# A load order in a fused attention and feed-forward kernel: the second batch's keys ahead of the third tile's queries

## The chip, the cores and the metric

The kernel runs on one core of a Trainium2 chip (trn2). The metric is the device time of one execution in microseconds (us). Before the change it is 861.98 us, the median of 3 runs (861.78 to 862.18).

The engines of the core are named as in the profile: PE is the matrix engine (PEld its weight loads), DVE the vector engine, ACT the scalar engine, POOL the GpSimd engine, and SP the engine that in this kernel issues every DMA. The engines run their own instruction streams and wait for each other through semaphores. SPq in a row is the time in which SP's sequencer issues a DMA; the transfer itself then runs on the core's 16 DMA engines.

## The reference

Three stages follow each other: attention over pooled keys and values, a gated feed-forward layer with RMS normalization, and a second feed-forward layer.

```python
# q, k, v: batch 4, heads 8, sequence 576, head_dim 64
k_p = k.reshape(B, H, Sp, 8, D).mean(axis=3)          # Sp = 576 / 8 = 72
v_p = v.reshape(B, H, Sp, 8, D).mean(axis=3)
scores = (1 / sqrt(D)) * q @ k_p^T
attn = softmax(scores)
x = (attn @ v_p), heads side by side                  # 2304 tokens x 512
xn = x / sqrt(mean(x * x) + 1e-6) * rms_g
h = silu(xn @ w_gate) * (xn @ w_val)                  # 512 x 1536 each
y = h @ w_out                                         # 1536 x 512
z = silu(y @ w2_in) @ w2_out                          # 512 x 2048, 2048 x 512
```

## The kernel before

The 2304 tokens are 18 tiles of 128. The attention stage goes through them one by one; it ends in the profile at about 90 us. The rest of the time belongs to the two feed-forward layers, whose products are built from split operands; the change touches nothing there.

Keys and values of one batch (8 heads, 72 pooled positions each, so 576 rows) are loaded whole, pooled by sums of 8 and then used by the four or five tiles of that batch. The batches begin in tiles 0, 4, 9 and 13. Queries are loaded tile by tile.

Names that the change and the prediction touch:

- `load_kv(b, kind)` (line 526) issues the load of batch b's keys (kind 0) or values (kind 1) into the buffer `kv`. For b = 1, kind 0 it waits for nothing and issues two DMAs: four chunks of 128 rows (L545, 1024 KB) and the last 64 rows (L547, 128 KB). Below these are k1 and k1's tail; v0 and v1 are the values of batches 0 and 1. A part of v1 goes out first (L536).
- `load_q(n)` (line 549) issues the load of tile n's queries into `qs[:, n % 2]` (L554, 256 KB, in pieces of 64 numbers). From n = 2 on it first waits until PE has transposed tile n - 2, whose buffer it takes. Below, q0, q1, q2, ... are these loads and tiles.
- `load_q(1)` stands inside `load_kv(0, 1)`, and `load_q(4)` inside `load_kv(1, 1)`.
- The vector `gT` (L697) holds rms_g; it is first used when tile 0 is normalized.

On PE, a list (`order`) written out by rules sets the sequence. In its step s it holds scores(s) (L1900), the transpose of the probabilities of tile s - 1 (prT, L1912), the transpose of the queries of tile s + 1 (L1887), from step 4 on the transpose of a finished x tile (L1944), where a batch begins with tile s + 1 the transpose of that batch's keys (L1878), and at last probabilities times values for tile s - 1 (pv, L1931). PE takes them strictly in that order: what waits holds all that is behind it.

The other engines feed it: POOL pools keys and values from batch 1 on (L830, L834, then L839 for keys into `ktwice`), DVE takes the maximum and subtracts it (L1478, L1483) and divides (L1505), ACT copies transposes out of PSUM (L1402 for queries, L1411 for probabilities, L1385 for keys) and takes exponentials (L1077). The transposed keys and the transposed probabilities share one region of PSUM, so the keys' transpose also waits until ACT has copied the probabilities of the tile before:

```python
def transpose_k(b):
    if b >= 1:
        pe.wait_ge(s_kTc, b)
    if first_tile[b] >= 1:
        pe.wait_ge(s_pTc, first_tile[b] - 1)
```

Before the attention PE does 30 transposes of an identity matrix (L2145), whose results nobody uses.

Of the kernel before, what the change touches and what calls it, by code (L numbers as in the profile page):

```python
# [20 lines left out]
def ffn_kernel(nc, q, k, v, w_gate, w_val, w_out, rms_g, w2_in, w2_out, out):  # L21
# [26 lines left out]
    def parts(n):  # L48
        at, found = n * P, []
        while at < (n + 1) * P:  # L50
            b = at // S
            end = min((b + 1) * S, (n + 1) * P)
            found.append((b, at - n * P, end - at))
            at = end
        return found
# [34 lines left out]
    for ph, (ffn, p) in enumerate(PHASES):  # L90
# [10 lines left out]
        if ph in ENDINGS:  # L101
# [26 lines left out]
                (BX, 1, 1, False), (BY, 2, 6, False), (BZ, 6, 2, False)]  # L128

    XORDER = [fx for _, _, fx, _ in PRODUCTS]  # L130

    def form_count(b, f):
# [50 lines left out]
    def esum(e, what, t):  # L183
# [3 lines left out]

    EHOME = [0, 1, 2, 0, 1, 3, 0]
    pieces = [EPART if fw < 3 else 1 for _, fw, _, _ in EPRODUCTS]
    e_load = [[16 * sum(pieces[m] * (e + (m <= i)) for m in range(NF) if EHOME[m] == EHOME[i]) for i in range(NF)]  # L190
              for e in range(2)]
# [14 lines left out]
    made += [("b", j) for j in range(2 * PART)]  # L206
    FOLD_AT = {("unit", first_unit[1] + 1 + j): ("b", j) for j in range(2 * PART)}
    f_pieces = [PART if fw < 3 else 1 for _, fw, _, _ in WPRODUCTS]
    f_load = [[16 * sum(f_pieces[m] * (e + (m <= i)) for m in range(i % 3, NF, 3)) for i in range(NF)] for e in range(2)]
    U2, N2 = first_unit[2], last_down[1] + 1  # L210
# [76 lines left out]
    with ctx:  # L287
# [237 lines left out]
        def _(sp):  # L525
            def load_kv(b, kind):
                if b >= 2:
                    sp.wait_ge((s_ksum, s_vsum)[kind], b - 1)
                if b == 2:
                    sp.wait_ge((s_kpartsum, s_vmidsum)[kind], (3, 1)[kind])  # L530
                rows_v, done, dst = (k_rows, v_rows)[kind], (s_k, s_v)[kind][b % 2], KV[b % 2][kind]
                full, c0 = (RC - 1) * P, 0
                if (b, kind) == (1, 1):

                    c0 = VPARTS[0][1]
                    sp.dma_start(dst[:, 0:c0, :], rows_v[b, 0:c0 * P, :].rearrange("(c p) x -> p c x", p=P))\  # L536
                      .then_inc(s_v1front, 16)
                    load_q(4)
                for i, (lo, hi) in enumerate((KPARTS[:2], VPARTS[:1])[kind] if b == 0 else []):
                    sp.dma_start(dst[:, lo:hi, :], rows_v[b, lo * P:hi * P, :].rearrange("(c p) x -> p c x", p=P))\  # L540
                      .then_inc(s_vfront if kind else s_kpart[i], 16)
                    c0 = hi
                if (b, kind) == (0, 1):
                    load_q(1)
                sp.dma_start(dst[:, c0:RC - 1, :],  # L545
                             rows_v[b, c0 * P:full, :].rearrange("(c p) x -> p c x", p=P)).then_inc(done, 16)
                sp.dma_start(dst[0:LAST, RC - 1, :], rows_v[b, full:R, :]).then_inc(done, 16)  # L547

            def load_q(n):
                if n >= 2:  # L550
                    sp.wait_ge(s_qTm, n - 1)
                for b, r0, m in parts(n):
                    s0 = n * P + r0 - b * S
                    sp.dma_start(qs[r0:r0 + m, n % 2, :, :],  # L554
                                 q[b, :, s0:s0 + m, :].rearrange("h s d -> s h d")).then_inc(s_q[n % 2], 16)
# [136 lines left out]
            load_kv(0, 0)  # L692
            load_q(0)
            load_kv(0, 1)
            load_q(2)
            load_kv(1, 0)
            sp.dma_start(gT[:, :], rms_g.rearrange("(c p) -> p c", p=P), allow_slow_non_contiguous=True)\  # L697
              .then_inc(s_g, 16)
            load_q(3)
# [1496 lines left out]
```

## Time and profile before

| | |
|---|---|
| median of 3 runs | 861.98 us (861.78 to 862.18) |
| profiled execution, its own time | 862.45 us |
| span of the instructions in it | 860.7 us |
| PE busy | 850.8 us, 99% of the span |
| DVE, POOL, ACT busy | 551.4, 421.2, 360.0 us |
| chain that ended last | PE 96%, DMA 2%, POOL 1% |

The profiled execution is 0.47 us above the median and lasts 1.7 us longer than its span. All times inside the trace count from the span's start. The engines' busy times overlap, so only what PE waits for, or what follows its last product, can set the end. The DMA share in a table of windows is the mean of 16 engines and can pass 1 where packets overlap.

### The profile page before, as it was taken

The page shows a single profiled execution, that of the slowest core. Times are in us where ns is not written, and L with a number is a line of the kernel's source. Part 1 is how long each engine was busy: PE and PEld are TensorE (multiplying, and loading weights), DVE is VectorE, ACT ScalarE, POOL GpSimd, SP SyncE. Part 2 cuts the span into 40 slices and gives each one's busy share as a digit, 9 for nine tenths or more (in the row PEclk, how much of TensorE's full clock was granted, in tenths as well). Part 3 has the DMA queues.
Part 4 walks back from the last instruction along what each step waited for, and adds up shares of the span by engine and source line. Part 5 has one row for each costly group of instructions (what it writes and reads, how often), then busy time and mean ns, then how long its engine had stood idle before and what let it go on. Part 6 is the DMA issues. An engine that isn't in the chain of part 4 may idle for free.

```text
span 860.7 us, 13899 instructions
## 1 busy us (share of the span) xinstructions
PE 850.8 (99%) x5292; PEld 830.6 (96%) x5292; DVE 551.4 (64%) x835; ACT 360.0 (42%) x640; POOL 421.2 (49%) x415
## 2 busy tenths in 40 slices
PE   7999999999999999999999999999999999999998
PEld 6999999999999999999899899999999999999998
DVE  6689757875545579955664345569634798335873
ACT  3689845543221325545553221324333444134521
POOL 6898999883427480577763044380161700004300
PEclk9999999999999999999999999999999999999999
DMA  9971578778869987565779489997789748687762
GB/s 255 269 218 42 221 262 318 271 303 311 326 223 407 407 329 266 200 260 223 278 292 370 160 294 362 356 400 262 268 287 361 252 189 286 250 330 253 253 238 102
DMA packets 94801, 235.78 MB, mean 274 GB/s; under 512 B 23056, under 2 KB 69136, under 8 KB 83216
## 3 DMA queue, kind: packets, MB, share of 16 engines
q1 hardware_dynamic: 94736, 234.90, 75.9%
q8 instruction: 42, 0.69, 0.3%
q14 instruction: 23, 0.19, 0.1%
HBM read 164.10 MB, written 70.78 MB: 273 GB/s over the span
## 4 chain that ended last, share of the span: by engine, by line
PE 96%; DMA 2%; POOL 1%; DVE 0%; SPq 0%; issue 0%; DVEq 0%; POOLq 0%
PE ps L2001 17%; PE ps L2003 17%; PE ps L2002 17%; PE ps L2139 5%; PE ps L2138 5%; PE ps L2137 5%; PE ps L2099 3%; PE ps L2097 3%; PE ps L2098 3%; PE ps L1931 3%; PE ps L2068 3%; PE ps L2069 3%; PE ps L2067 3%; PE ps L2044 2%; PE ps L2043 2%; PE ps L2042 2%
## 5 line engine op out<-in xcount | busy, mean ns | idle before, releaser
L2001 PE MATMUL ps<-xh,wr 128*128 128x384 f32 x840 | 282.9, 337 | 0.3
L2003 PE MATMUL ps<-xh,wr 128*128 128x384 f32 x840 | 281.3, 335 | 0.0
L2002 PE MATMUL ps<-xl,wr 128*128 128x384 f32 x840 | 281.0, 335 | 0.0
L2001 PEld LDWEIGHTS ps<-xh,wr 128*128 128x128 f32 x840 | 157.6, 188 | 4.4 <-DVE qt L1570 1.5
L2002 PEld LDWEIGHTS ps<-xl,wr 128*128 128x128 f32 x840 | 157.8, 188 | 0.3
L2003 PEld LDWEIGHTS ps<-xh,wr 128*128 128x128 f32 x840 | 157.7, 188 | 0.0
L2138 PE MATMUL ps<-ew,efh 128*128 128x256 f32 x336 | 95.1, 283 | 0.0
L2139 PE MATMUL ps<-ew,efl 128*128 128x256 f32 x336 | 95.1, 283 | 0.0
L2137 PE MATMUL ps<-ew,efh 128*128 128x256 f32 x336 | 95.1, 283 | 0.0
L1589 DVE TENSOR_TENSOR qt<-ps,qt 128x384 f32<-128x384 f32 x84 | 46.4, 556 | 49.8 <-PE ps L2003 49.7
L950 POOL TENSOR_TENSOR eh<-eh 128x768 f32<-128x768 f32 x8 | 17.2, 2168 | 122.8 <-DVE efl L1666 122.8
L2139 PEld LDWEIGHTS ps<-ew,efl 128*128 128x128 f32 x336 | 64.5, 192 | 0.0
L2138 PEld LDWEIGHTS ps<-ew,efh 128*128 128x128 f32 x336 | 64.5, 192 | 0.0
L2137 PEld LDWEIGHTS ps<-ew,efh 128*128 128x128 f32 x336 | 64.5, 192 | 0.0
L1179 ACT ACTIVATE qt<-ps 128x384 f32<-128x384 f32 x42 | 20.6, 492 | 101.7 <-PE ps L2003 101.2
L1666 DVE TENSOR_TENSOR efl<-eh,efh 128x768 fp32r<-128x768 f32 x56 | 59.8, 1123 | 5.1 <-ACT efh L1279 5.1
L930 POOL TENSOR_TENSOR ebt<-raw_z 128x256 f32<-128x256 f32 x8 | 5.9, 739 | 112.4 <-PE ps L2099 40.0
L1279 ACT ACTIVATE efh<-eh 128x768 fp32r<-128x768 f32 x56 | 43.0, 835 | 41.2 <-PE ps L2139 41.2
L2097 PE MATMUL ps<-fh,fw 128*128 128x384 f32 x168 | 56.1, 334 | 0.0
L2098 PE MATMUL ps<-fl,fw 128*128 128x384 f32 x168 | 56.1, 334 | 0.0
L2099 PE MATMUL ps<-fh,fw 128*128 128x384 f32 x168 | 56.1, 334 | 0.0
L1578 DVE TENSOR_TENSOR qt<-ps,qt 128x384 f32<-128x384 f32 x42 | 23.4, 557 | 51.0 <-PE ps L2003 51.0
(198 smaller groups left out, 1767.1 us busy)
## 6 DMA issues: line engine op xcount, KB each, us to landing
wr<-ring_home SPq DMA_DIRECT2D x40, 1792.0 KB, 9.7
ring_home<-wr SPq DMA_DIRECT2D x20, 1792.0 KB, 8.0
ew<-ending_home SPq DMA_DIRECT2D x8, 2048.0 KB, 8.5
out_home<-wo SPq DMA_DIRECT2D x14, 1024.0 KB, 9.4
fw<-fold_home SPq DMA_DIRECT2D x8, 1536.0 KB, 7.8
ew<-out_home SPq DMA_DIRECT2D x24, 512.0 KB, 7.2
fw<-out_home SPq DMA_DIRECT2D x18, 512.0 KB, 6.6
ending_home<-eb SPq DMA_DIRECT2D x16, 512.0 KB, 10.8
```

What stands on the lines that cost most here:

```text
L1279: act.activation(efh[e][i % 2][:, 2 * j:2 * j + 2, :], ending_part(f, j), ACT.Copy).then_inc(s_ehi, 1)
L1589: dve.tensor_tensor(done if units[u][1] == "V" else qt[:, c, :], done, tiles(u)[:, c, :], ALU.add)\
L1666: dve.tensor_tensor(efl[e][i % 2][:, 2 * j:2 * j + 2, :], ending_part(f, j), efh[e][i % 2][:, 2 * j:2 * j + 2, :], ALU.subtract).then_inc( ...
L2001: pe.matmul(out_ps, w_hi, x_hi, start=first and c == 0, stop=False, skip_group_check=True)
L2002: pe.matmul(out_ps, w_hi, x_lo, start=False, stop=False, skip_group_check=True)
L2003: ins = pe.matmul(out_ps, w_lo, x_hi, start=False, stop=c == 1, skip_group_check=True)
L2097: pe.matmul(out_ps, w_hi, h_hi, start=first and c == 0, stop=False, skip_group_check=True)
L2098: pe.matmul(out_ps, w_hi, h_lo, start=False, stop=False, skip_group_check=True)
L2099: ins = pe.matmul(out_ps, w_lo, h_hi, start=False, stop=c == 2 * PART - 1, skip_group_check=True)
L2137: pe.matmul(out_ps, h_hi, w_hi, start=first and c == 0, stop=False, skip_group_check=True)
L2138: pe.matmul(out_ps, h_hi, w_lo, start=False, stop=False, skip_group_check=True)
L2139: ins = pe.matmul(out_ps, h_lo, w_hi, start=False, stop=c == 2 * EPART - 1, skip_group_check=True)
```

## The change

Two lines of SP's program trade places: k1 and its tail are issued before q2, where they were issued behind it.

```diff
             load_kv(0, 0)
             load_q(0)
             load_kv(0, 1)
+            load_kv(1, 0)
             load_q(2)
-            load_kv(1, 0)
             sp.dma_start(gT[:, :], rms_g.rearrange("(c p) -> p c", p=P), allow_slow_non_contiguous=True)\
               .then_inc(s_g, 16)
             load_q(3)
```

SP's instructions from the start of the program to q3, before (without a line) or after (with +) the change. `kv<-in_k 128x4x512` is k1, the `64x512` behind it its tail, the `qs<-in_q` that moves is q2, and the last one is q3. `qT_made` is the count of query tiles that PE has transposed.

```order
 L545 DMA kv<-in_v 128x2x512
 L547 DMA kv<-in_v 64x512
-L554 DMA qs<-in_q 128x8x64 [waits qT_made]
 L545 DMA kv<-in_k 128x4x512
 L547 DMA kv<-in_k 64x512
+L554 DMA qs<-in_q 128x8x64 [waits qT_made]
 L697 DMA gT<-in_moe_rms_g 128x4x1
 L554 DMA qs<-in_q 128x8x64 [waits qT_made]
```

The two loads of k1 no longer stand behind the wait for PE's first transpose of queries; q2 now stands behind both of them. Everything from gT on keeps its place.

PE's instructions around the use of q2, the same in both kernels; `q_loaded0` on the second L1887 row is q2's arrival.

```order
L1912 MATMUL ps<-ident,pr 128x128 [waits kT_copied,kT_pr_cleared,exp_made]
L1912 MATMUL ps<-ident,pr 128x128 x4
L1887 MATMUL ps<-ident,qs 128x128 [waits qT_copied,q_loaded0]
L1887 MATMUL ps<-ident,qs 128x128 x3
L1931 MATMUL ps<-vb0,prT 128x130 [waits v0_front_blocks_made,v_blocks_made,prT_copied]
```

Nothing moves on PE, DVE, ACT or POOL. Behind q2's transpose PE holds pv of tile 0 and then the scores of tile 2.

## Rows read from the trace of the kernel before

**Rows 1.** The page: busy us (share of the span) and count, by engine.
```profile
PE 850.8 (99%) x5292; PEld 830.6 (96%) x5292; DVE 551.4 (64%) x835; ACT 360.0 (42%) x640; POOL 421.2 (49%) x415
```

**Rows 2.** Windows, PE alone: stretch, its length, busy (count), clock, DMA share, GB/s.
```profile
0.00:25.00 25.00, 18.73 (x127) 1.00 1.06 253
25.00:840.00 815.00, 814.20 (x5019) 1.00 0.77 279
```

**Rows 3.** Waits of PE over the whole span: us in total, times, longest.
```profile
PE ps L1900 <- DVE pr L1483: 1.3, 1, 1.3
PE ps L1931 <- ACT prT L1411: 1.2, 2, 0.8
PE ps L1878 <- POOL ktwice L839: 0.5, 1, 0.5
```

**Rows 4.** Timeline of PE, 14.5 to 25 us: start, duration, instruction, [idle before <-releaser].
```profile
14.57 0.71 PE L1912 MATMUL ps<-ident,pr 128*128 128x128 f32 x5
15.12 0.60 PE L1887 MATMUL ps<-ident,qs 128*128 128x128 f32 x4
16.55 1.74 PE L1931 MATMUL ps<-vb,prT 128*128 128x130 f32 x12 [0.84 <-ACT prT L1411]
18.13 1.20 PE L1900 MATMUL ps<-kT,qT 128*128 128x144 f32 x8
...
19.71 0.60 PE L1887 MATMUL ps<-ident,qs 128*128 128x128 f32 x4
...
24.91 0.30 PE L1878 MATMUL ps<-ident,ktwice 128*128 128x128 f32 x1 [0.46 <-POOL ktwice L839]
```

**Rows 5.** Chain of waits, in order of time, 29 to 31 us.
```profile
29.52 0.44 PE ps L1887 x4
```

**Rows 6.** Timeline of SP's issues, 9 to 16 us: q2, k1, its tail, q3, q4.
```profile
9.11 0.38 SPq L554 DMA_DIRECT2D qs<-in_q  x1
9.53 0.58 SPq L545 DMA_DIRECT2D kv<-in_k  x1
10.15 0.52 SPq L547 DMA_DIRECT2D kv<-in_k  x1
...
12.25 0.98 SPq L554 DMA_DIRECT2D qs<-in_q  x1
...
15.75 2.32 SPq L554 DMA_DIRECT2D qs<-in_q  x2
```

**Rows 7.** DMAs issued 9.05 to 12 us: count, KB, us from issue to landing.
```profile
kv<-in_k SPq DMA_DIRECT2D x1, 1024.0 KB, 7.8
qs<-in_q SPq DMA_DIRECT2D x1, 256.0 KB, 5.4
kv<-in_k SPq DMA_DIRECT2D x1, 128.0 KB, 8.2
gT<-in_moe_rms_g SPq DMA_DIRECT2D x1, 2.0 KB, 7.9
```

**Rows 8.** The same, issued 12.2 to 13.2 us (q3).
```profile
qs<-in_q SPq DMA_DIRECT2D x1, 256.0 KB, 7.3
```

**Rows 9.** The same for v0's tail, issued at 7.31 us.
```profile
kv<-in_v SPq DMA_DIRECT2D x1, 128.0 KB, 6.3
```

**Rows 10.** Timeline of POOL and ACT, 18 to 25 us.
```profile
18.50 3.04 POOL L830 TENSOR_TENSOR kv<-kv 128x512 f32<-128x512 f32 x2 [3.07 <-DMA kv<-in_k]
...
23.23 1.54 POOL L839 TENSOR_TENSOR ktwice<-kv 128x640 f32<-128x640 f32 x1
...
24.05 0.70 ACT L1411 ACTIVATE prT<-ps 128x640 f32<-128x640 f32 x1 [1.77 <-PE ps L1912]
```

**Rows 11.** Windows, PE alone: identity transposes of the start, then the end.
```profile
1.60:4.70 3.10, 3.04 (x14) 1.00 0.87 264
857.00:858.00 1.00, 0.83 (x7) 1.00 0.02 4
859.00:860.00 1.00, 0.00 (x0) 0.90 0.70 262
```

## The prediction

> **What bounds the kernel now.** I read the page first: PE is busy for 850.8 of 860.7 us [rows 1]. Then PE's busy time by windows: of the first 25 us it works 18.73, so 6.3 are idle; from 25 to 840 us it works 814.20 of 815, so 0.8 are idle [rows 2]. Two things follow. Whatever PE loses in the first 25 us has no idle time behind it to be made good in, and comes out at the end one for one. And nothing outside the first 25 us can be gained by moving a load. The waits of PE [rows 3] show what the early idle time is made of: the longest are for DVE's subtraction before the second tile's scores (1.3 us), for ACT's copy of the probabilities (1.2 us in two) and, once, 0.5 us for `ktwice`, which is POOL's pooled k1. That last one is the only wait in the list that the moved load feeds.
>
> **What is removed: the wait for k1.** POOL starts on k1 at 18.50 after 3.07 us without work, released by the DMA, and ends `ktwice` at 23.23 + 1.54 = 24.77; PE takes it at 24.91 [rows 4, 10]. k1 lands earlier after the change, so that wait looks like 0.46 us to be had. It isn't: the keys' transpose also needs the shared PSUM region, which is free when ACT has copied the probabilities, at 24.05 + 0.70 = 24.75 [rows 10]. That is 0.02 us before POOL. With k1 any amount earlier the keys' transpose still starts 0.02 us earlier at most. I count the gain as 0.
>
> **What is moved: q2.** Landing times before, issue plus time to landing [rows 6, 7, 8, 9]:
>
> - v0's tail 7.31 + 6.3 = 13.6
> - q2 9.11 + 5.4 = 14.5
> - k1 9.53 + 7.8 = 17.3
> - k1's tail 10.15 + 8.2 = 18.4 (the same number read at POOL: work begins at 18.50)
> - gT 10.71 + 7.9 = 18.6, and q3 12.25 + 7.3 = 19.6
>
> (gT's issue is 10.15 + 0.52 and a gap of 0.04.) They land in the order of issue, each some 5 to 8 us after it, with the DMA share at 1.06 over the first 25 us [rows 2]. So this is one full queue, and a transfer lands when everything ahead of it has been moved. PE needs q2 at 15.12, 0.6 us after it lands [rows 4].
>
> After the change SP issues k1 as soon as v0's tail is out, from about 7.8, and its two issues (0.58 and 0.52) end near 9.0, about when the wait before q2 is met anyway. q2 is issued at 9.1 to 9.2 as before, but behind 1152 KB. When it lands can be bounded from rows:
>
> - Low end: take only k1's own time behind q2, 17.3 - 14.5 = 2.8, and let the tail cost its share of the bytes, an eighth of that, 0.35. q2 lands at 14.5 + 2.8 + 0.35 = 17.65.
> - High end, and the value I take: before, the queue had finished q2, k1 and the tail together at 18.4. It holds the same three afterwards, with q2 last. Since the queue isn't empty before them, the last of the three lands when the last of them did, at 18.4 (18.36). I take this end because it needs nothing but the sum of the same work, while the other assumes that a tail is cheap, and the row shows it landing 1.1 us behind k1.
>
> PE, then: it ends prT of tile 0 near 15.3, comes to q2's transpose at 15.12 and now finds it at 18.36 + 0.04 = 18.40. The transposes take 0.44 until the next work can follow [rows 5], so pv of tile 0 starts at 18.84. Before, it started at 16.55, having itself waited 0.84 us [rows 4]. That wait is the cover: of the 3.28 us that q2 is late, 1.43 - 0.44 = 0.99 vanish in it, and 2.29 stay. The break-even is q2 usable at 16.55 - 0.44 = 16.1. By the low end the loss is 17.69 - 16.11 = 1.6 us.
>
> From pv on, the pattern repeats as before, all shifted: scores of tile 2 at 18.13 + 2.29, the next waits for ACT's copy hang on PE's own prT and shift with it, and so does the copy that frees the region for the keys, to 24.75 + 2.29 = 27.0. `ktwice` is by then long made (k1's tail lands about 0.9 earlier, the time q2 took behind v0's tail, 14.5 - 13.6). So the 0.46 us before the keys' transpose stays too, now wholly ACT's.
>
> **What hangs on the later transpose of q2.** q4's issue waits for it, and v1's rest, q5 and k2 stand behind q4 on SP. Before, q4 went out at 15.75 [rows 6]; now at about 19.0. q3 and the front of v1 are issued already, and the queue then still holds v1's front (512 KB, roughly 2 us behind q3's 19.6), so q4 arrives in the queue while it is still busy, or within half a microsecond of it. q4 is wanted at about 23.9 + 2.3 = 26.2. q3 lands at 19.6 as before and is now wanted at 19.71 + 2.29 = 22.0, v1 ten microseconds later. Cost 0. gT is wanted only by tile 0's normalization near 30 us. Cost 0.
>
> **Sum.** 862.45 (the profiled execution) + 2.3 = 864.75; that execution is 0.47 above the median of the runs, so for the timed runs 861.98 + 2.3 = 864.3 us. With the low end it is 863.6.
>
> The Trainium skill bears on the size. Its page "DMA: Bandwidth & Descriptors", section "Anatomy of one DMA", gives the moving time of a transfer as bytes over 436 GB/s beside a fixed part. By it k1 and its tail (1.18 MB) would hold q2 for an estimated 2.7 us, q2 would be there at 17.2 and the loss would be 1.1 us, 863.1 in all. The trace disagrees: from q2's landing to the tail's are 3.9 us, at 300 GB/s.
>
> **Rivals.**
>
> *The clock falls (865.8).* PE would stand idle from about 15.3 to 18.4, 3.1 us. The longest gaps before are 1.3 us [rows 3], and the granted clock stays at full speed, 2.4 GHz, through them. At the end of the program PE stops at about 857.8 and the granted clock falls inside 859 to 860, two microseconds later: the mean of 0.90 is a fifth of that window at 0.5, 1.2 GHz [rows 11]. So it can fall within some 2 us of a stop. What it costs: the first identity transposes go at 3.04 / 14 = 0.217 us each, against 0.44 / 4 = 0.11 at full speed [rows 5, 11], for at least the 3.0 us of that window. Three microseconds at half speed lose 1.5, which gives 864.3 + 1.5 = 865.8; up to the 6.7 us between the first transpose and q0 at 8.4 they would lose 3.4. Against it: the gap before the end differs, nothing at all follows there, and here PE is dense up to it. The Trainium skill, page "TensorE: Matmul & The Clock Gate", Part 1, likewise has the clock gated to half after an idle time; the trace's end agrees, and whether it does so in this gap no row says.
>
> *q2's lateness is cheaper (about 863.1).* The three transfers share the engines rather than follow each other, or the earlier issue of k1 fills holes, and q2 is there by 17.2: a loss of 1.1. For it: DMA share above 1, packets overlap. Against it: the strict order of the landings above.
>
> *Not slower (862.0).* If q2's small pieces passed k1 in the queue it would be usable before 16.1, the cover of 0.84 plus the slack of 0.6 would swallow the delay, and the result is the old time less 0.02. The point from which it decides is that 16.1. A real gain isn't in the rows: all of k1's wait is 0.46, and ACT's copy holds it. Also in this case belongs that SP's order doesn't become the queue's order. The landings speak against it.
>
> **Chances.** Forecast (2.3 lost, clock full) 0.48; clock falls 0.26; cheaper 0.16; not slower 0.10, of which 0.02 for a gain from somewhere that I don't see. The predicted time is 864.3. The range must take in the cheaper case and the middle of the clock case: 862.6 to 866.2, which leaves out the not-slower case and the upper half of the clock's cost, together under 0.2. About 0.2%, 1.7 us, is what can be told from no change here, so slower means above 863.7. Of the forecast's 0.48 about 0.05 lies below that (the low end of q2's landing), and nearly all of the cheaper case does. That gives slower 0.70, same 0.28, faster 0.02.
>
> **What the profile would show.** Right: SP's rows with k1 at about 7.8 and q2 at about 9.1; q2 landing 9 us after its issue; PE waiting about 3 us for `qs` before the third L1887 group; no or hardly any wait charged to pv of tile 0; POOL starting on k1 near 17.5; all of PE's starts from there on 2.3 us later, with the keys' transpose at 27.2. Wrong: k1 and q2 landing together or q2 first; PE's L1887 for q2 before 16.1; a granted clock below 1.00 between 15 and 25 us, with transposes at 0.22 us each (the first rival); or a PE that catches up between 25 and 840 us, which would mean that its busy time there hides waits.

## The result and the profile after

The changed kernel takes 865.86 us (median of 6 runs, 865.40 to 866.73); the kernel before, run beside it, 862.24 (6 runs, 861.78 to 863.30). The ratio is 1.0047, with a 95% interval of 1.0037 to 1.0057: slower by 3 to 5 us. The forecast was 864.3, with a range of 862.6 to 866.2. The direction is the one forecast and the measured time lies inside the range, but the loss is 3.6 us by the medians and 4.1 by the ratio, and not 2.3. The number of the first rival, a falling clock, was 865.8.

The profiled execution takes 865.82 us with a span of 864.1, against 862.45 and 860.7: 3.4 us more in both.

The page after, busy us by engine and (second line) the granted clock in 40 slices, answers to [rows 1]:

```profile
PE 851.2 (99%) x5292; PEld 831.5 (96%) x5292; DVE 551.6 (64%) x835; ACT 359.8 (42%) x640; POOL 422.3 (49%) x415
...
PEclk9999999999999999999999999999999999999999
```

Here nothing is to be seen: the work is the same, and a slice is 21.6 us long, too coarse for the place. The windows show it. Each row gives stretch, length, PE busy (count), granted clock, DMA share and GB/s of the kernel after; the first two answer to [rows 2]:

```profile
0.00:25.00 25.00, 15.97 (x100) 0.93 0.89 242
25.00:840.00 815.00, 814.08 (x5019) 1.00 0.76 278
...
17.00:18.00 1.00, 0.00 (x0) 1.00 0.87 130
18.00:19.00 1.00, 0.67 (x4) 0.77 0.27 40
19.00:20.00 1.00, 1.00 (x6) 0.50 1.02 395
20.00:21.00 1.00, 1.00 (x6) 0.50 0.42 145
21.00:22.00 1.00, 1.00 (x7) 0.53 0.70 160
22.00:23.00 1.00, 1.00 (x10) 1.00 0.79 133
```

All of the loss is made in the first 25 us, where PE works 15.97 us instead of 18.73; behind them it is as dense as before. And the granted clock, which in the kernel before is 1.00 in each of these windows, stands at 0.50 (1.2 GHz) from about 18.54 to about 21.94: 0.46 + 1 + 1 + 0.94 = 3.4 us by the four means, if it is one stretch.

PE's timeline after, against [rows 4]:

```profile
8.70 0.66 PE L1887 MATMUL ps<-ident,qs 128*128 128x128 f32 x4 [2.00 <-DMA qs<-in_q]
...
14.56 0.71 PE L1912 MATMUL ps<-ident,pr 128*128 128x128 f32 x5
18.33 0.97 PE L1887 MATMUL ps<-ident,qs 128*128 128x128 f32 x4 [3.06 <-DMA qs<-in_q]
19.09 3.06 PE L1931 MATMUL ps<-vb,prT 128*128 128x130 f32 x12
21.99 1.20 PE L1900 MATMUL ps<-kT,qT 128*128 128x144 f32 x8
23.02 0.71 PE L1912 MATMUL ps<-ident,pr 128*128 128x128 f32 x5
...
27.17 0.71 PE L1912 MATMUL ps<-ident,pr 128*128 128x128 f32 x5
27.71 0.60 PE L1887 MATMUL ps<-ident,qs 128*128 128x128 f32 x4
28.72 0.74 PE L1878 MATMUL ps<-ident,ktwice 128*128 128x128 f32 x5 [0.41 <-issue]
```

The transposes of the probabilities start at 14.56, as before (14.57). q2's transpose starts at 18.33 after 3.06 us without work. The twelve products of pv, 1.74 us before, take 3.06: they, and the end of q2's transposes, run at half clock. The clock did not fall while PE stood idle. It fell at about 18.54, 0.2 us after PE had begun to work again, and stayed low while PE worked without a gap. The scores of tile 2 start 21.99 - 18.13 = 3.86 us late, and the keys' transpose 28.72 - 24.91 = 3.81. The wait in front of the keys is still there (0.41 instead of 0.46), although it is no longer charged to POOL. The first line is the wait for q0: 2.00 us in this execution, 0.94 in the profiled one of before, and the clock stayed at 1.00 behind it.

SP's issues after, against [rows 6], and then the landings of k1, its tail and q2 (answers to [rows 7]; each row is from its own stretch of issues):

```profile
7.73 0.49 SPq L547 DMA_DIRECT2D kv<-in_v  x1
8.26 0.59 SPq L545 DMA_DIRECT2D kv<-in_k  x1
8.89 0.83 SPq L547 DMA_DIRECT2D kv<-in_k  x1
9.76 0.59 SPq L554 DMA_DIRECT2D qs<-in_q  x1
```

```profile
kv<-in_k SPq DMA_DIRECT2D x1, 1024.0 KB, 7.3
kv<-in_k SPq DMA_DIRECT2D x1, 128.0 KB, 8.6
...
qs<-in_q SPq DMA_DIRECT2D x1, 256.0 KB, 8.5
```

k1 lands at 8.26 + 7.3 = 15.6, its tail at 8.89 + 8.6 = 17.5, q2 at 9.76 + 8.5 = 18.26. The last of the three lands within 0.1 us of where the last of them landed before (18.36). SP issued q2 at 9.76 and not at the 9.1 to 9.2 that was forecast.

### The profile page after: what moved, and what is told of

The parts are those of the page before. It is cut to its first block, busy times and chain, and to the rows that moved or that the text cites. A ratio compares the mean times of both kernels' runs of the same rounds, so it can differ in the third digit from the quotient of the medians.

```text
span 864.1 us, 13899 instructions
## 1 busy us (share of the span) xinstructions
PE 851.2 (99%) x5292; PEld 831.5 (96%) x5292; DVE 551.6 (64%) x835; ACT 359.8 (42%) x640; POOL 422.3 (49%) x415
## 4 chain that ended last, share of the span: by engine, by line
PE 97%; DMA 1%; SPq 1%; DVE 0%; issue 0%; ACT 0%; DVEq 0%
PE ps L2001 17%; PE ps L2003 17%; PE ps L2002 17%; PE ps L2139 5%; PE ps L2138 5%; PE ps L2137 5%; PE ps L1931 4%; PE ps L2099 3%; PE ps L2098 3%; PE ps L2097 3%; PE ps L2068 3%; PE ps L2069 3%; PE ps L2067 3%; PE ps L1900 2%; PE ps L2044 2%; PE ps L2042 2%
```

## The experiments

After the result the theory (A in the expectations) was: q2's place in the queue costs 2.2 us, and the idle time that it makes lets the clock fall, which costs 1.6 more. This is worked out from the profiles. With the clock full, the scores of tile 2 follow the start of q2's transposes by 0.44 and the time of pv, 18.13 - 16.55 = 1.58. So they would start at 18.33 + 2.02 = 20.35, which is 2.2 us late, and they did start at 21.99, which is 1.64 more. The rivals were that the second part comes of something on ACT or DVE (theory B), that the queue works otherwise, and that k1's wait could have been had. All ratios below are to the kernel before, run in the same rounds.

**Filling PE's idle time (e1, 24 transposes).** The order of the changed kernel, and on PE 24 transposes of the identity matrix that nobody reads:

```diff
             for what, n in order:
+                if (what, n) == ("q", 2):
+                    for _ in range(24):
+                        pe.transpose(ps[:, 7, 0:P], ident[:, :], ident[:, :])
                 if what == "q":
```

> The changed order, with 24 more transposes of the identity on PE in front of q2's transpose, into a PSUM bank that pv of tile 0 starts anew; nobody reads them. They take 24 x 0.11 = 2.6 us of the 3.06 us for which PE waits there. Theory A (the lateness of q2 costs 2.3 and the fallen clock 1.5): the granted clock stays at 1.00 between 18 and 22, q2's transpose still starts near 18.33, pv of tile 0 near 18.8, the scores of tile 2 near 20.4 instead of 21.99, and the kernel takes 1.5 us less than the changed one, about 2 us over the one before (ratio 1.0025). Theory B (the 1.5 us are not the clock's but come of something else that q2's wait sets off on ACT or DVE): the scores of tile 2 stay near 22 and the time within 0.3 us of the changed kernel's.

Measured: 863.86 us (10 runs, 862.94 to 864.50), ratio 1.0024 (1.0015 to 1.0034), and no run had a clock below full. PE's timeline, then windows:

```profile
15.12 2.78 PE L2149 MATMUL ps<-ident 128*128 128x128 f32 x24
18.17 0.66 PE L1887 MATMUL ps<-ident,qs 128*128 128x128 f32 x4 [0.26 <-DMA qs<-in_q]
18.66 1.67 PE L1931 MATMUL ps<-vb,prT 128*128 128x130 f32 x12
20.16 1.20 PE L1900 MATMUL ps<-kT,qT 128*128 128x144 f32 x8
```

```profile
14.00:18.00 4.00, 3.91 (x36) 1.00 1.36 228
18.00:22.00 4.00, 3.83 (x32) 1.00 0.65 196
```

q2 is as late as in the changed kernel, but pv takes 1.67 us and the scores start at 20.16, 2.03 late instead of 3.86. More work on PE made the kernel faster than the changed one was in the result (ratio 1.0047, 1.0037 to 1.0057); of the two theories only A says so. What is left, 0.24% or 2.1 us, is q2's lateness by itself.

**Filling part of it (e2, 12 transposes).** The same edit with 12.

> The same with 12 transposes, 1.3 us: PE's idle time before q2 shrinks to about 1.75 us. Theory A: PE idled 1.3 us in the kernel before and 2.0 before q0 in the changed one without a fall of the clock, so the clock stays at 1.00 in most or all runs and the time equals that with 24. If it is the total idle time in the neighbourhood that counts and 1.75 is still too long, the clock falls in part or all of the runs and the time lies up to 1.5 us higher. Theory B: no change from the changed kernel.

Measured: 864.13 us (8 runs, 863.26 to 866.14), ratio 1.0028 (1.0018 to 1.0038). In the profile PE waits 1.72 us for q2 and the clock is full:

```profile
14.72 1.47 PE L2149 MATMUL ps<-ident 128*128 128x128 f32 x12
17.91 0.66 PE L1887 MATMUL ps<-ident,qs 128*128 128x128 f32 x4 [1.72 <-DMA qs<-in_q]
18.40 1.67 PE L1931 MATMUL ps<-vb,prT 128*128 128x130 f32 x12
```

Seven runs lie between 863.26 and 864.52 with a mean clock of 1.000 over the span; the eighth took 866.14 with 0.998. A mean lower by 0.002 over 864 us is 1.7 us of clock, or some 3.4 us spent at half. So the fall doesn't seem to be a fixed property of a program: here it came in one run of eight. That run has no trace, so its fall is read from the mean clock and the time, and its place isn't shown; the same holds for every unprofiled run below.

**Half of k1 ahead of q2 (e3).** The old order, with two of k1's four chunks issued first under a semaphore of their own, for which POOL waits too:

```diff
             load_kv(0, 1)
+            sp.dma_start(KV[1][0][:, 0:2, :], k_rows[1, 0:2 * P, :].rearrange("(c p) x -> p c x", p=P))\
+              .then_inc(s_k1front, 16)
             load_q(2)
             load_kv(1, 0)
```

These lines are SP's; `load_kv(1, 0)` now begins with chunk 2.

> The order of the kernel before, except that only the first two of k1's four chunks (512 KB) are issued ahead of q2; the other two and the tail follow q2. Theory A (a full queue served in order, q2 free to land until 16.1): q2 lands about 1.4 us later than before, at 15.9, PE starts q2's transpose near 15.95 and pv of tile 0 at 16.5, as before; clock 1.00; time within 0.3 us of the kernel before. Rival (each KB ahead of q2 costs PE its time, without cover): 1.4 us slower. Rival (the queue isn't served in order): q2 lands as before, at 14.5.

Measured: 862.03 us (11 runs), ratio 1.0003 (0.9994 to 1.0012). PE's timeline (this kernel's lines stand 6 higher):

```profile
15.93 0.66 PE L1893 MATMUL ps<-ident,qs 128*128 128x128 f32 x4 [0.78 <-DMA qs<-in_q]
16.50 1.74 PE L1937 MATMUL ps<-vb,prT 128*128 128x130 f32 x12
18.08 1.20 PE L1906 MATMUL ps<-kT,qT 128*128 128x144 f32 x8
```

PE takes q2 at 15.93 (forecast 15.95) and pv starts at 16.50, as before. PE's new wait of 0.78 us for q2 costs nothing, since pv would have waited anyway. In this execution POOL does hold the keys' transpose, though: PE waits 0.62 us for `ktwice`, and from the transposes of the probabilities to the keys' it takes 25.03 - 23.26 = 1.77 us instead of 1.60. k1's tail landed at 10.16 + 8.3 = 18.5, no earlier than before, while PE was 0.13 us ahead. So the two holders of that wait are close enough to change places.

**Three quarters of k1 ahead (e5).** The same edit with three chunks.

> As with half of k1 ahead of q2, but three of its four chunks (768 KB) go ahead and the fourth and the tail follow. Theory A (order of the queue, cover until 16.1, clock): by 2.8 us for the four chunks, q2 lands 2.1 later than before, at 16.6; PE takes it at 16.65 after an idle time of about 1.4 us, pv of tile 0 starts at 17.1 instead of 16.55, 0.55 us late, the clock stays at 1.00, and the kernel takes 0.5 us more than the one before (ratio 1.0006). Rival (the cost comes in one step, when the clock falls): the same time as before or 2 us more.

Measured: 862.27 us (11 runs, 861.57 to 865.05), ratio 1.0009 (1.0000 to 1.0017).

```profile
12.96 1.22 PE L1906 MATMUL ps<-kT,qT 128*128 128x144 f32 x8 [1.30 <-DVE pr L1489]
14.01 0.71 PE L1918 MATMUL ps<-ident,pr 128*128 128x128 f32 x5
16.25 0.66 PE L1893 MATMUL ps<-ident,qs 128*128 128x128 f32 x4 [1.53 <-DMA qs<-in_q]
16.74 1.67 PE L1937 MATMUL ps<-vb,prT 128*128 128x130 f32 x12
```

This execution runs 0.56 us ahead of the profiled one of before from the start (probabilities transposed at 14.01 against 14.57), so pv's 16.74 stands for 17.30: 0.75 late, against a forecast of 0.55. The timed runs alone can't tell this from no loss, as the interval reaches 1.0000; the trace shows it. Nine runs lie at 861.57 to 862.88, with a clock of 1.000; two, at 864.37 and 865.05, have 0.998. The cost begins at the break-even, as in theory A, and in some runs the clock seems to add its own on top.

**Only the tail ahead (e6).** k1's tail before `load_q(2)`, the four chunks behind it.

> The kernel before with only k1's tail (128 KB, 64 rows) ahead of q2, and the four chunks behind it. It tells what the tail costs in the queue. By its share of the bytes: q2 lands 0.35 us later than before, at about 14.85. By the distance at which tails land behind what they follow: 1.06 us later, at 15.6. In both cases PE has it before 16.1 and the time is that of the kernel before.

Measured: 861.73 us (10 runs), ratio 1.0001 (0.9991 to 1.0010). q2 lands at 14.66. This execution runs 0.56 us ahead of the profiled one of before, so that stands for 15.2, between the two numbers forecast (14.85 and 15.6). The table gives how long after v0's tail q2 lands, a distance that doesn't depend on how the execution began, for the nine profiled executions (landings to 0.1 us).

| ahead of q2 | v0's tail lands | q2 lands | distance | more than before |
|---|---|---|---|---|
| nothing (before) | 7.31 + 6.3 | 9.11 + 5.4 | 0.9 | |
| nothing (e4, below) | 6.78 + 6.1 | 8.69 + 5.3 | 1.1 | 0.2 |
| tail, 128 KB (e6) | 6.92 + 6.2 | 8.76 + 5.9 | 1.5 | 0.6 |
| 512 KB (e3) | 7.18 + 6.4 | 9.03 + 6.9 | 2.4 | 1.5 |
| 768 KB (e5) | 6.88 + 6.2 | 8.71 + 7.5 | 3.1 | 2.2 |
| 1152 KB (after) | 7.73 + 5.9 | 9.76 + 8.5 | 4.6 | 3.7 |
| 1152 KB (e1) | 7.23 + 6.4 | 9.46 + 8.7 | 4.5 | 3.6 |
| 1152 KB (e2) | 7.01 + 6.2 | 9.23 + 8.6 | 4.6 | 3.7 |
| 1152 KB (e7, below) | 7.07 + 6.4 | 9.36 + 9.2 | 5.1 | 4.2 |

512 KB cost 1.5 us and 256 more cost 0.8, so four chunks would come to about 3.0 (not run alone); with the tail's 0.6 that makes 3.6, and the four executions with all of it ahead gave 3.6 to 4.2. So a queue in order, priced by what stands ahead of q2, describes them. The small terms are weak: two executions of the same order differ by 0.2, so the tail's price is 0.4 to 0.6, near its share of the bytes. And the price holds for the sum, not for each transfer: k1's own four chunks landed 1.9, 2.0, 2.7 and 3.0 us behind v0's tail (after, e1, e2, e7), while q2 kept to 4.5 to 5.1.

**POOL ready earlier (e4).** The kernel before, with POOL's first sum over k1 left out, so that batch 1's pooled keys are wrong but early:

```diff
-                pool_pairs(1, kind, 0, 2)
+                if kind == 1:
+                    pool_pairs(1, kind, 0, 2)
```

> The kernel before, with POOL leaving out the first of its sums over k1 (chunks 0 and 1, 1.5 us), so the pooled keys of batch 1 are wrong there but ready 1.5 us earlier, near 23.3 instead of 24.77. Theory A (the copy of the probabilities by ACT, which ends at 24.75, holds the keys' transpose anyway): the transpose starts at 24.9 as before, the wait of about 0.46 us is now charged to something other than POOL, and the time is within 0.2 us of the kernel before. Rival (the wait is POOL's): the transpose starts at 24.46 and the kernel is 0.4 us faster.

Measured: 861.56 us (11 runs), ratio 0.9999 (0.9990 to 1.0008). POOL, PE and ACT around the keys' transpose:

```profile
21.48 1.54 POOL L839 TENSOR_TENSOR ktwice<-kv 128x640 f32<-128x640 f32 x1
...
22.62 0.71 PE L1913 MATMUL ps<-ident,pr 128*128 128x128 f32 x5
...
23.37 0.70 ACT L1412 ACTIVATE prT<-ps 128x640 f32<-128x640 f32 x1 [1.70 <-PE ps L1913]
...
24.17 0.74 PE L1879 MATMUL ps<-ident,ktwice 128*128 128x128 f32 x5 [0.40 <-issue]
```

`ktwice` is done at 23.02, more than a microsecond before PE comes for it, and the wait is still 0.40. PE starts 0.10 after ACT's copy ends at 24.07. From the transposes of the probabilities to the keys' it takes 24.17 - 22.62 = 1.55 us, before 24.91 - 23.31 = 1.60 (23.31 is that transpose's start in the timeline before). So 0.05 of the 0.46 was POOL's. In e5 and e6 the profile itself charges this wait, 0.40 us, to ACT's copy.

**The changed kernel once more (e7).**

> The changed kernel once more, unaltered, for a comparison on the same chip and in the same rounds as the other two, and to see in how many runs the clock falls. If the fall is what sets it apart from the filled ones, every run that shows a clock below full has the longer time: about 3.9 us over the kernel before, against 2.1 to 2.4 with the filled ones.

Measured: 865.11 us (5 runs), ratio 1.0034 (1.0021 to 1.0046). The runs fall in two groups:

| run | us | mean clock |
|---|---|---|
| 1 | 866.02 | 0.998 |
| 2 | 865.16 | 0.998 |
| 3 | 865.11 | 0.998 |
| 4 | 863.40 | 1.000 |
| 5 | 864.18 | 1.000 |

The same program is 1.6 us faster in the two runs in which the clock stayed up (863.8 against 865.4 in the mean), and these two stand 2.0 us over the 861.82 of the kernel before, about as the filled kernels do. In all 6 runs of the result the mean clock is lower (0.996 to 0.998). The expectation held that every run with a lower clock is among the longer ones: 3.6 us over the kernel before, for 3.9 forecast. The profiled run is one with the fall. PE's timeline and the windows give

```profile
18.58 0.66 PE L1887 MATMUL ps<-ident,qs 128*128 128x128 f32 x4 [3.47 <-DMA qs<-in_q]
19.07 3.02 PE L1931 MATMUL ps<-vb,prT 128*128 128x130 f32 x12
```

```profile
14.00:18.00 4.00, 1.11 (x10) 1.00 1.25 239
18.00:22.00 4.00, 3.42 (x17) 0.65 0.86 216
22.00:25.00 3.00, 2.64 (x20) 0.90 0.86 242
```

The means 0.65 and 0.90 are 2.8 and 0.6 us at half, 3.4 again, from about 19.2 on: 0.6 us after PE had taken up its work.

## Why the prediction was wrong, step by step

**The step that failed** is the clock's term, which the sum put at nothing: the forecast took "clock full" (0.48) over the first rival, "the clock falls" (0.26). The runs showed a fall that costs 1.64 us in the trace and 1.6 between the two groups of e7, by the mean clock in 9 of the 11 runs of this kernel. The gap was rightly foreseen (3.1 us, measured 3.06), and so was the possibility. I set the row at the end of the program aside because the work around it differs, and leaned on the gaps of 1.3 us, which say nothing of one more than twice as long. (They were not the longest either: PE stood for 1.66 us before its first transpose, and rows 3 leave that and the 0.94 us for q0 out.)

Nor would the end of the program have given a rule, since the changed kernel idled that long twice with the clock full: 2.00 us before q0, and at the end, where PE stops at 861.16:

```profile
862.00:863.00 1.00, 0.00 (x0) 1.00 0.52 199
863.00:864.00 1.00, 0.00 (x0) 1.00 0.17 64
```

What the rows before allowed was to call a gap of 3.1 us untested, and to price the fall as part of the likely case.

**The price of the fall** was taken as half of the 3.0 us for which the first transposes ran slow, 1.5. The stretch at half clock was 3.4 us. That the two are close is luck: the 3.0 us were the length of the stretch that was read, and the granted clock in that row is 1.00 although a transpose took 0.217 us, so the row records no fall. The rival's 865.8 is nearer to the median than its parts are to theirs, too: 2.3 + 1.5 = 3.8, where the trace has 2.2 + 1.6 - 0.4 = 3.4.

**q2's landing**: forecast 18.36 by "the last of the three lands when the last of them did", measured 18.26, and 18.56 in e7. The choice of that end over 17.65 held. What I said against the other end, that tails are dear, did not hold well: e6 puts the tail at 0.4 to 0.6 us, nearer to the 0.35 of its bytes than to the 1.1 of its distance. The four chunks were dearer than their 2.8, about 3.0 by e3 and e5.

**The cover in front of pv**: break-even 16.1. e3 (usable at 15.93, no loss at pv), e5 (0.75 late for 16.81 in the time of before) and e1 (2.03 late for 18.17) lie on one line behind it. For the changed kernel it gives 18.33 + 0.44 + 1.58 - 18.13 = 2.2 us, forecast 2.29.

**k1's wait worth nothing**: right. POOL had `ktwice` at 22.32 + 1.55 = 23.87 in the changed kernel (forecast 23.9), the wait stayed at 0.41, and e4 shows the same without touching a DMA.

**Nothing lost through q4, v1, q5**: right; PE waits for no `qs` after q2. SP's list of issues shows q4 leaving at 19.33, when q2's transpose, from 18.33 for 0.97 us, lets it.

**"One for one to the end"** was nearly right. Of 3.81 us at the keys' transpose 3.4 arrive. PE's windows of 60 to 75 and of 500 to 600 us, before and then after, show where some came back: PE waits 0.17 and 0.15 us less there than before.

```profile
60.00:75.00 15.00, 14.54 (x121) 1.00 0.53 151
500.00:600.00 100.00, 99.85 (x573) 1.00 0.96 348
```

```profile
60.00:75.00 15.00, 14.71 (x121) 1.00 0.57 161
500.00:600.00 100.00, 100.00 (x575) 1.00 0.95 344
```

**The sum.** 2.2 (q2) + 1.6 (clock) - 0.4 (given back) = 3.4, for 3.4 in the spans.

**The page's rule of moving time** (the Trainium skill, "DMA: Bandwidth & Descriptors", "Anatomy of one DMA") would have put k1 and its tail at an estimated 2.7 us; the page gives it for transfers that GpSimd issues, and SP issues these. The table says 3.6 to 4.2 us here, so the measurement decides. The rule of the Trainium skill that an idle matrix engine loses its clock ("TensorE: Matmul & The Clock Gate", Part 1) was the one to give more weight. Both traces of the changed kernel agree with it: the clock stands at 0.50 behind gaps of 3.06 and 3.47 us, and in the first it stays at 1.00 behind the 2.00 us before q0.

## What to carry to other kernels

A load that is wanted later but issued earlier held back what stood behind it by its whole transfer time here, where the queue was full. Before moving it, list for each transfer behind it when it lands and when it is wanted; here q2 had 1.6 us to spare and was given 3.6 to 4.2 more. And where the moved wait opens a gap on the matrix engine longer than any in the trace, price the fall of the clock as part of the likely case, and use a few idle products in the gap as the test for it.

A wait charged to one engine is not gained by making that engine early: look for what else ends within a tenth of a microsecond of it.

## What the runs showed of the hardware

The fall of the clock isn't the same in every execution of one program. Counting a mean clock of 0.998 or less as a fall, it came in 9 of 11 runs of the changed kernel (PE idle for 3.06 and 3.47 us in the two profiled ones), in 1 of 8 with 1.72 us (e2), in 2 of 11 with 1.53 us (e5), and in none of 11 and 10 with 0.78 and 0.26 us (e3, e1). In the two traces that have it, the clock fell 0.2 and 0.6 us after PE had begun to work again, and the low stretch was 3.4 us long in both. It cost the run 1.6 to 2.5 us (means with and without it: e7 865.4 and 863.8, e2 866.1 and 864.0, e5 864.7 and 862.2). What decides between two runs of one program stays open.
